# Count tables with an operand in PSUM, and the last combines divided between VectorE and GpSimd, in an attention and mixture-of-experts kernel

## The chip, the cores and the metric

The kernel runs as one program on one core of a Trainium2 chip. The metric is the device time of one execution in microseconds (us); lower is better. The engines are TensorE (PE in the rows, its weight loads PEld), VectorE (DVE), ScalarE (ACT), GpSimd (POOL) and SyncE (SP), each with an instruction stream of its own. A "q" behind an engine's name (ACTq, DVEq, POOLq) is its queue, which issues DMAs and handles registers and semaphores.

## What is computed

```python
scores = scale * np.matmul(q, k.transpose(0, 1, 3, 2))     # 2 x 8 heads, 768 tokens, 64 wide
keep = is_sink | in_window                                  # 4 sinks, window of 128
a = softmax(np.where(keep, scores, -1e9))
x = merge_heads(np.matmul(a, v))                            # 1536 tokens x 512
h = x @ w_in                                                # 512 x 2048
x = (h - np.tanh(h)) @ w_out                                # 2048 x 512
noisy = x @ w_gate + np.log1p(np.exp(x @ w_noise)) * noise  # 8 experts
for each token: the two experts with the highest noisy value, softmax of the two as weights
for e in range(8):
    out[mask] += weight * (np.maximum(x[mask] @ w1[e], 0.0) @ w2[e])   # 512 x 1024, 1024 x 512
```

All of it is float32. Every matmul of the three stages behind the attention is made of three: each operand is split into a high part rounded to fp32r and a low part, the remainder, and hi*hi + hi*lo + lo*hi are added up in PSUM.

## The kernel before, in words

**Stages.** The first 94 us or so are attention. Then four blocks of 384 tokens go through the dense layer, and VectorE computes the routing of each block while TensorE works on the next. A token's row is scattered by GpSimd (an indirect DMA) into `sorted_x`, grouped by expert. The expert stage then works on `TILES` = 31 tiles of 128 sorted rows, expert by expert. With these inputs 29 tiles hold rows; the last two are spare and are computed all the same.

**One tile of the expert stage.** TensorE's loop for tile t does `up(t)` (24 matmuls of 512 columns, L1598), `turn_rows(t + 1)` (four transposes of the next tile's rows, L1580) and `down(t - 2)` (24 matmuls, L1630). The hidden rows of a tile go by DMA to memory and back (`hid_out`, `hid_in`, L901 and L909, both issued by ScalarE) so that VectorE can transpose them in 32x32 blocks (`turn_hidden`, L1199). VectorE's loop does, for tile t: `relu_out(t)` (L1207), `rows_turned_out(t + 1)` (L1190, the low part of the next tile's turned rows), `turn_hidden(t - 1)`, `result_out(t - 2)` (L1214, the result from PSUM to `ys`), and `hid_turned_out(t - 1)` (L1220). ScalarE does `relu_out(t)`, `hid_out(t)`, the high part of the turned rows (L886), the load of rows t + 2, `hid_turned_out(t - 1)` (L922), `store_rows(t - 2)` (L926, `ys` to `sorted_y`) and `hid_in(t)`. The order is written out by hand. On each engine an instruction that waits holds up all behind it.

**The tables.** While the first tiles run, VectorE computes small tables from the counts of rows per expert. Each step is `link`ed: it is followed by a wait of VectorE for its own result. The tables are in the `arena` (SBUF) or, those called `..._t`, in bank 6 of PSUM. The last of them, `stores_i` (L1334 to L1345), tells GpSimd how many tiles must be stored before the rows of a block can be gathered. It stands between `hid_turned_out(2)` and the loop over tiles 4 to 28. It reads `placed`, the running counts after each block, which `route_place` writes (L1143).

**The weights.** SyncE loads the weights of an expert in four pieces into a ring of two slots, when TensorE is done with the expert that was there. GpSimd splits each piece into the high part (L656) and the low part (L658), 128 x 2048 elements per instruction.

**The end.** When all experts are split, GpSimd gathers for each of the 12 output tiles of 128 tokens first the rows of one expert (`gathered_a`), and scales them by the gate (L740), then those of the other expert (`gathered_b`). These are multiplied by their gate (L745) and added (L748) in `combine`. The first gather of each block of three tiles waits for the stores that it needs (L757 to L759); gather i waits for gather i - 3. SyncE stores each output tile when it is combined (L603), and waits at the end for these stores and for those of `sorted_y` (L606). On TensorE the last pieces are `down(29)` and `down(30)`; VectorE takes out result 29 (L1366), ScalarE result 30 (L986).

The waits behind which the last tiles' results stand:

```python
            for i in range(TT):
                sp.wait_ge(summed, i + 1)
                sp.dma_start(out[token(i):token(i) + P, :], gathered_a[:, i, :]).then_inc(out_stored, 16)
            sp.wait_ge(out_stored, 16 * TT)

            sp.wait_ge(ys_stored, 16 * TILES)
```

## Time and profile before

| | |
|---|---|
| median of 3 runs | 769.12 us (768.66 to 769.92) |
| the profiled execution's own time | 771.69 us |
| its span, first to last instruction | 769.9 us |
| granted TensorE clock, mean | 0.978 |
| TensorE matmul busy | 741.4 us (96%) |
| GpSimd busy | 464.2 us (60%) |
| VectorE busy | 364.6 us (47%) |
| ScalarE busy | 229.4 us (30%) |

Times in the rows are microseconds from the start of the span. The chain of waits follows the work that ended last back to its start. A clock of 1.00 is TensorE's full 2.4 GHz, 0.50 is 1.2 GHz.

### The profile page before, as it was taken

How to read it: one execution, taken by the hardware profiler on the slowest of the kernel's cores; microseconds unless marked ns; L12 is line 12 of the kernel's file. 1: busy time of each engine (PE TensorE's matmuls, PEld its weight loads, DVE VectorE, ACT ScalarE, POOL GpSimd, SP SyncE). 2: the span in 40 equal slices, each digit the busy share in tenths (PEclk: the TensorE clock that was granted, in tenths of full speed). 3: DMA queues.
4: the chain of work that ended last, by engine and by line, in shares of the span. 5: the costliest groups of instructions: out<-in, count | busy, mean ns of one | idle time of the engine just before them, and what ended most of it. 6: DMA issues, size and time to landing. Idle time of an engine off the chain costs nothing.

```text
span 769.9 us, 12878 instructions
## 1 busy us (share of the span) xinstructions
PE 741.4 (96%) x3892; PEld 622.4 (81%) x3893; DVE 364.6 (47%) x877; ACT 229.4 (30%) x528; POOL 464.2 (60%) x264
## 2 busy tenths in 40 slices
PE   7999999999999999999999699999999999999993
PEld 5777899898989998998877478888888888888882
DVE  4777544224423532353464854454454454455440
ACT  5999622223222322322221111211211211212220
POOL 6888997000300110038959936858885899987687
PEclk8999999999999999999899989999999999999997
DMA  8642483000200010025633548677776777867664
GB/s 298 231 139 92 144 314 150 0 1 1 83 1 0 14 68 0 0 73 186 238 146 107 179 152 260 216 235 261 241 247 214 249 256 246 257 192 247 225 199 150
DMA packets 59550, 121.46 MB, mean 158 GB/s; under 512 B 7040, under 2 KB 21504, under 8 KB 59520
## 3 DMA queue, kind: packets, MB, share of 16 engines
q1 hardware_dynamic: 28512, 63.92, 24.3%
q10 hardware_dynamic: 27168, 44.57, 17.2%
q0 software_dynamic: 3840, 12.59, 5.0%
q8 instruction: 16, 0.26, 0.1%
q14 instruction: 14, 0.11, 0.0%
HBM read 81.74 MB, written 39.32 MB: 157 GB/s over the span
## 4 chain that ended last, share of the span: by engine, by line
PE 90%; POOL 3%; DVE 2%; issue 1%; DMA 1%; ACT 1%; POOLq 0%; ACTq 0%; DVEq 0%
PE bank L1598 21%; PE bank L1630 20%; PE bank L1455 18%; PE bank L1505 18%; PE bank L1408 4%; PE bank L1399 3%; PE bank L1381 3%; PE bank L1580 2%; PE bank L1521 1%; POOL gathered_b L745 1%; POOL gathered_a L748 1%; POOL gathered_b L733 1%; PE bank L1515 1%; DMA hid_lanes<-hid_by_lane 1%; DVE arena L1334 0%
## 5 line engine op out<-in xcount | busy, mean ns | idle before, releaser
L704 POOL DMA_INDIRECT sorted_x<-y_rows,arena x24 | 24.2, 1010 | 208.9 <-DVEq L1142 202.8
L658 POOL TENSOR_TENSOR ring<-ring_raw,ring 128x2048 fp32r<-128x2048 f32 x32 | 148.0, 4624 | 2.5
L1630 PE MATMUL bank<-ring,hidT_hi 128*128 (+1 forms) x464 | 148.2, 400 | 1.0 <-DVE hidT_lo L1220 1.0
L656 POOL TENSOR_TENSOR ring<-ring_raw,ones 128x2048 fp32r<-128x2048 f32 x32 | 115.9, 3622 | 54.3 <-DMA ring_raw<-in_moe_w 54.3
L1598 PE MATMUL bank<-ring,xsT_hi 128*128 (+1 forms) x496 | 137.8, 401 | 10.8 <-DVE xsT_lo L1190 8.8
L1598 PEld LDWEIGHTS bank<-ring,xsT_hi 128*128 128x128 f32 x496 | 95.5, 194 | 32.8 <-issue 12.2
L1505 PE MATMUL bank<-w_out_sb,gated_hi 128*128 128x512 f32 x384 | 121.2, 397 | 0.0
L1630 PEld LDWEIGHTS bank<-ring,hidT_hi 128*128 128x128 f32 x464 | 84.9, 188 | 19.6 <-issue 1.2
L1630 PE MATMUL bank<-ring,hidT_lo 128*128 (+1 forms) x232 | 91.6, 395 | 0.0
L1063 DVE TENSOR_TENSOR arena<-bank,arena 128x384 f32<-128x384 f32 x64 | 35.7, 557 | 113.7 <-ACT arena L835 112.7
L1455 PE MATMUL bank<-xT_hi,w_in_hi 128*128 (+1 forms) x256 | 87.0, 340 | 0.0
L1455 PE MATMUL bank<-xT_hi,w_in_lo 128*128 (+1 forms) x256 | 86.4, 338 | 0.0
L1455 PE MATMUL bank<-xT_lo,w_in_hi 128*128 (+1 forms) x256 | 86.0, 336 | 0.0
L1505 PEld LDWEIGHTS bank<-w_out_sb,gated_hi 128*128 128x128 f32 x384 | 70.9, 188 | 12.3
L1598 PE MATMUL bank<-ring,xsT_lo 128*128 (+1 forms) x248 | 78.4, 398 | 0.0
L1505 PE MATMUL bank<-w_out_sb,gated_lo 128*128 128x512 f32 x192 | 75.9, 395 | 0.0
L835 ACT ACTIVATE arena<-bank 128x384 f32<-128x384 f32 x64 | 31.4, 491 | 139.8 <-PE bank L1455 139.8
L1207 DVE TENSOR_SCALAR hid<-bank 128x512 f32<-128x512 f32 x31 | 21.4, 691 | 97.3 <-PE bank L1598 97.3
L922 ACT CAST hidT_hi<-bank 128x512 fp32r<-128x512 f32 x58 | 31.5, 590 | 117.9 <-PE bank L1630 97.5
L1199 DVE STREAM_TRANSPOSE bank<-hid_lanes 128x512 f32<-128x512 f32 x56 | 64.5, 1197 | 2.2 <-DMA hid_lanes<-hid_by_lane 2.2
L1067 DVE TENSOR_TENSOR gated_lo<-arena,gated_hi 128x384 fp32r<-128x384 f32 x64 | 45.8, 716 | 40.0 <-ACT gated_hi L840 40.0
L1598 PEld LDWEIGHTS bank<-ring,xsT_lo 128*128 128x128 f32 x248 | 47.7, 192 | 10.4
(201 smaller groups left out, 1074.1 us busy)
## 6 DMA issues: line engine op xcount, KB each, us to landing
ring_raw<-in_moe_w SPq DMA_DIRECT2D x48, 512.0 KB, 4.2
hid_by_lane<-hid ACTq DMA_DIRECT2D x28, 512.0 KB, 3.4
hid_lanes<-hid_by_lane ACTq DMA_DIRECT2D x28, 512.0 KB, 4.5
ring_raw<-in_moe_w SPq DMA_DIRECT2D x8, 1024.0 KB, 7.0
sorted_y<-ys ACTq DMA_DIRECT2D x31, 256.0 KB, 2.6
xs<-sorted_x ACTq DMA_DIRECT2D x27, 256.0 KB, 3.7
sorted_y<-zeros SPq DMA_DIRECT2D x1, 4864.0 KB, 25.5
arena<-in_k SPq DMA_DIRECT2D x8, 520.0 KB, 4.1
```

The source lines that it names most:

```text
L656: pool.tensor_tensor(hi, raw, one_like(raw), ALU.mult).then_inc(rounded, 1)
L658: ins = pool.tensor_tensor(lo, raw, hi.bitcast(F32), ALU.subtract)
L835: act.activation(tanh_h[fc % 2][:, :], bank[fc % 2][:, 0:BLK], ACT.Tanh).then_inc(tanh_ready, 1)
L922: act.copy(hidT_hi[b][:, half * BANK:(half + 1) * BANK], bank[3 + half][:, :]).then_inc(hidT_rounded, 1)
L1063: dve.tensor_tensor(gated[fc % 2][:, :], bank[fc % 2][:, 0:BLK], tanh_h[fc % 2][:, :], ALU.subtract).then_inc(gated_ready, 1)
L1067: dve.tensor_tensor(gated_lo[fc % G][:, :], gated[fc % 2][:, :], gated_hi[fc % G][:, :].bitcast(F32), ALU.subtract).then_inc(gated_split, 1)
L1199: dve.transpose(bank[3 + half][:, :].rearrange("p (c i g) -> p g c i", c=EC // 2, g=QUAD), lane_blocks[:, :, half * (EC // 2):(half + 1) * ...
L1408: last = pe.matmul(attn_bank[half][D * u:D * u + D, at:at + w], lhs, rhs, start=start, stop=stop, skip_group_check=True)
L1455: last = pe.matmul(bank[fc % 2][:, 0:BLK], w[:, at:at + P], x[:, bass.ds(blk * CH + c, 1), :].rearrange("p a s -> p (a s)"), start=c == 0 ...
L1505: last = pe.matmul(bank[2 + kk][:, :], g[fc % G][:, kk * P:(kk + 1) * P], w_out_sb[:, fc, w, :], start=fc == 0 and n == 0, stop=fc == FC - ...
L1598: last = pe.matmul(bank[1 + half][:, :], x[:, c * P:(c + 1) * P], ring[:, bass.ds(at * 2 * WE + (w + c * FE + half * BANK), BANK)], start= ...
L1630: last = pe.matmul(bank[5 + b][:, :], x[:, c * P:(c + 1) * P], ring[:, bass.ds(at * 2 * WE + (w + CH * FE + c * DM), DM)], start=c == 0 an ...
```

## The change

It has three parts.

1. **The table of stores.** `placed` is first copied into PSUM (`placed_all_t`). `placed_d`, and `placed_end`, lie in PSUM now (`placed_d_t`, `placed_end_t`). So no instruction of this table reads two operands from SBUF, and none goes from SBUF to SBUF with a single operand. In `route_place`, `placed` is written by an addition with an operand in PSUM, three instructions earlier than the copy that it replaces.
2. **The last combines.** GpSimd combines output tiles 0 to 5. VectorE combines tiles 6 to 11, behind all its other work, with one instruction for each (multiply by the gate and add). SyncE waits for a new semaphore for these six. GpSimd still issues all the gathers.
3. **The last results.** ScalarE takes out result 29 as well as result 30.

```diff
+    LATE = 2 * KB
...
             for i in range(TT):
-                sp.wait_ge(summed, i + 1)
+                if i < TT - LATE:
+                    sp.wait_ge(summed, i + 1)
+                else:
+                    sp.wait_ge(last_summed, i + 1 - (TT - LATE))
...
                     for i in range(blk * KB, blk * KB + KB):
                         gather(kk, rows, i)
-                        if i >= 2:
-                            finish(i - 2)
-                for i in range(TT - 2, TT):
-                    finish(i)
+                        if kk == 0 and i >= 2:
+                            scale(i - 2)
+                        if kk == 1 and 2 <= i < TT - LATE + 2:
+                            combine(i - 2)
+                if kk == 0:
+                    scale(TT - 2)
+                    scale(TT - 1)
...
             hid_turned_out(TILES - 1, used=TILES - 1, b=1)
+            result_out(TILES - 2)
             store_rows(TILES - 2)
 
-            act.wait_ge(expert_done, TILES + 1)
-            act.wait_ge(ys_stored, 16 * (TILES - 1))
-            act.copy(ys[:, :], bank[6][:, :]).then_inc(ys_ready, 1)
+            result_out(TILES - 1, b=1)
             store_rows(TILES - 1)
...
+                dve.tensor_tensor(placed[:, bass.ds(blk, 1), :].rearrange("p b e -> p (b e)"), carry[:, KB - 1, :],
+                                  bank[7][:, 2 * P + (KB - 1) * E:2 * P + KB * E], ALU.add)
                 link(dve.tensor_tensor(row_t, rank_t, carry[:, 0:KB, :], ALU.add))
...
-                dve.tensor_copy(placed[:, bass.ds(blk, 1), :].rearrange("p b e -> p (b e)"), carry[:, KB, :])
                 link(dve.tensor_copy(carry[:, 0, :], carry[:, KB, :]))
...
-            link(dve.tensor_tensor(placed_swap[:, :, :], placed[:, :, :],
+            link(dve.tensor_copy(placed_all_t, placed[:, :, :]))
+            link(dve.tensor_tensor(placed_swap[:, :, :], placed_all_t,
                                    swap[:, None, :].to_broadcast([P, NBLK, E]), ALU.mult))
-            link(dve.tensor_reduce(placed_d[:, :], placed_swap[:, :, :], AX.X, ALU.add))
+            link(dve.tensor_reduce(placed_d_t, placed_swap[:, :, :], AX.X, ALU.add))
             link(dve.tensor_tensor(placed_at_t, swap[:, None, E - TOP:E].to_broadcast([P, NBLK, TOP]),
-                                   placed_d[:, :, None].to_broadcast([P, NBLK, TOP]), ALU.mult))
+                                   placed_d_t[:, :, None].to_broadcast([P, NBLK, TOP]), ALU.mult))
...
-            link(dve.tensor_tensor(placed_end[:, :, :], placed_tiles[:, :, :],
+            link(dve.tensor_tensor(placed_end_t, placed_tiles[:, :, :],
                                    tile_end_t[:, None, E - TOP - 1:E - 1].to_broadcast([P, NBLK, TOP]), ALU.add))
-            dve.tensor_scalar(stores_i[:, :, :], placed_end[:, :, :], 16.0, None, ALU.mult).then_inc(stores_known, 1)
+            dve.tensor_scalar(stores_i[:, :, :], placed_end_t, 16.0, None, ALU.mult).then_inc(stores_known, 1)
...
             hid_turned_out(TILES - 1, 1)
-            result_out(TILES - 2)
+
+
+            for i in range(TT - LATE, TT):
+                dve.wait_ge(gathered[1][i], 16)
+                dve.wait_ge(scaled, i + 1)
+                dve.scalar_tensor_tensor(gathered_a[:, i, :], gathered_b[:, i, :], gate_at[1][:, i:i + 1],
+                                         gathered_a[:, i, :], ALU.mult, ALU.add).then_inc(last_summed, 1)
```

Two places show how the instructions stand. The first is on VectorE, between the split of tile 2's turned hidden rows and the loop; `arena` is SBUF, `bank` is PSUM. Before:

```order
L1220 TENSOR_TENSOR hidT_lo<-bank,hidT_hi 128x512 x2
L1334 TENSOR_TENSOR arena<-arena 128x32
L1336 TENSOR_REDUCE arena<-arena 128x4
L1337 TENSOR_TENSOR bank<-arena 128x8
L1339 TENSOR_TENSOR bank<-arena,bank 128x8
L1340 TENSOR_SCALAR bank<-bank 128x8
L1341 TENSOR_SCALAR bank<-bank 128x8
L1342 CAST arena<-bank 128x8
L1343 TENSOR_TENSOR arena<-arena,bank 128x8
L1345 TENSOR_SCALAR arena<-arena 128x8
```

With the change:

```order
L1235 TENSOR_TENSOR hidT_lo<-bank,hidT_hi 128x512 x2
L1349 COPY bank<-arena 128x32
L1350 TENSOR_TENSOR arena<-bank,arena 128x32
L1352 TENSOR_REDUCE bank<-arena 128x4
L1353 TENSOR_TENSOR bank<-arena,bank 128x8
L1355 TENSOR_TENSOR bank<-arena,bank 128x8
L1356 TENSOR_SCALAR bank<-bank 128x8
L1357 TENSOR_SCALAR bank<-bank 128x8
L1358 CAST arena<-bank 128x8
L1359 TENSOR_TENSOR bank<-arena,bank 128x8
L1361 TENSOR_SCALAR arena<-bank 128x8
```

Nine instructions became ten, and in the three that had `arena` alone on both sides (L1334, L1337 and L1345) a `bank` stands now.

The second is on GpSimd at its end: the combine of output tile 4, then that of 5, with the last gathers. Before, the last rows of GpSimd are:

```order
L733 DMA gathered_b<-sorted_y,arena 128x512
L745 TENSOR_TENSOR gathered_b<-gathered_b,arena 128x512
L748 TENSOR_TENSOR gathered_a<-gathered_a,gathered_b 128x512
L745 TENSOR_TENSOR gathered_b<-gathered_b,arena 128x512
L748 TENSOR_TENSOR gathered_a<-gathered_a,gathered_b 128x512
L745 TENSOR_TENSOR gathered_b<-gathered_b,arena 128x512
L748 TENSOR_TENSOR gathered_a<-gathered_a,gathered_b 128x512
L76 UNCONDITIONAL_BRANCH
```

With the change:

```order
L751 TENSOR_TENSOR gathered_b<-gathered_b,arena 128x512
L754 TENSOR_TENSOR gathered_a<-gathered_a,gathered_b 128x512
L739 DMA gathered_b<-sorted_y,arena 128x512
L763 TENSOR_LOAD arena
L763 ISA x2
L739 DMA gathered_b<-sorted_y,arena 128x512 x3
L77 UNCONDITIONAL_BRANCH
```

The gathers of tiles 8 to 11 now follow one another, and twelve instructions of GpSimd (two for each of six tiles) are gone. In their place `L1387 SCALAR_TENSOR_TENSOR` stands six times at VectorE's end.

## Rows read from the trace of the kernel before

**Rows 1.** First lines of the page: the span.
```profile
span 769.9 us, 12878 instructions
```

**Rows 2.** Waits of PE from 440 us on: total, times, longest us.
```profile
PE bank L1598 <- DVE xsT_lo L1190: 8.4, 1, 8.4
```

**Rows 3.** Chain of waits, around 440 us: start us, us, what.
```profile
438.12 3.06 issue
...
443.97 8.52 PE bank L1598 x24
...
458.52 5.45 PE bank L1598 x24
```

**Rows 4.** DVE's timeline, 416 to 442 us: start, us, line, op, out<-in.
```profile
416.19 0.16 DVE L1314 TENSOR_SCALAR bank<-arena 128x12 f32<-128x12 f32 x1
...
429.26 3.89 DVE L1334 TENSOR_TENSOR arena<-arena 128x32 f32<-128x32 f32 x1
...
433.41 3.29 DVE L1337 TENSOR_TENSOR bank<-arena 128x8 f32<-128x8 f32 x1
...
437.75 3.52 DVE L1345 TENSOR_SCALAR arena<-arena 128x8 int32<-128x8 f32 x1
```

**Rows 5.** POOL's timeline, 412 to 476 us.
```profile
412.05 4.58 POOL L658 TENSOR_TENSOR ring<-ring_raw,ring 128x2048 fp32r<-128x2048 f32 x1
...
428.51 4.59 POOL L658 TENSOR_TENSOR ring<-ring_raw,ring 128x2048 fp32r<-128x2048 f32 x1
433.06 3.60 POOL L656 TENSOR_TENSOR ring<-ring_raw,ones 128x2048 fp32r<-128x2048 f32 x1
436.74 4.49 POOL L658 TENSOR_TENSOR ring<-ring_raw,ring 128x2048 fp32r<-128x2048 f32 x1
...
467.35 3.60 POOL L656 TENSOR_TENSOR ring<-ring_raw,ones 128x2048 fp32r<-128x2048 f32 x1 [17.88 <-DMA ring_raw<-in_moe_w]
```

**Rows 6.** Windows: us; PE, PEld, DVE, ACT, POOL busy (x); PEclk, DMA share, GB/s.
```profile
445.00:450.00 5.00, 5.00 (x13) 3.93 (x12) 2.62 (x4) 1.06 (x2) 4.46 (x1) 0.51 0.65 197
450.00:455.00 5.00, 5.00 (x25) 4.10 (x24) 1.09 (x2) 1.19 (x2) 0.00 (x0) 1.00 0.15 52
```

**Rows 7.** L909 (`hid_in`): the one of 429.0 us, then four from 415 to 470 us.
```profile
L909 ACTq DMA_DIRECT2D hid_lanes<-hid_by_lane x1: 326/326/326, 429.0 to 429.0; - x1
...
DMA to landing us min/median/max: 4.4/4.4/4.4
...
DMA to landing us min/median/max: 3.6/4.5/5.1
```

**Rows 8.** POOL's timeline from 716 us to its end.
```profile
717.55 0.95 POOL L733 DMA_INDIRECT gathered_b<-sorted_y,arena  x1 [0.30 <-issue]
...
739.73 0.99 POOL L733 DMA_INDIRECT gathered_b<-sorted_y,arena  x1 [1.81 <-DMA sorted_y<-ys]
...
743.31 0.99 POOL L733 DMA_INDIRECT gathered_b<-sorted_y,arena  x1
...
764.40 1.26 POOL L748 TENSOR_TENSOR gathered_a<-gathered_a,gathered_b 128x512 f32<-128x512 f32 x1
```

**Rows 9.** Landing times by line: L603 (12), L926 from 690 us (7), L733 from 700 us (17).
```profile
DMA to landing us min/median/max: 2.0/2.0/3.8
...
DMA to landing us min/median/max: 2.1/3.0/3.8
...
DMA to landing us min/median/max: 3.4/3.6/6.0
```

**Rows 10.** ACT's timeline at its end.
```profile
757.76 0.59 ACT L986 COPY ys<-bank 128x512 f32<-128x512 f32 x1 [6.97 <-PE bank L1630]
758.38 0.34 ACTq L926 DMA_DIRECT2D sorted_y<-ys  x1
```

**Rows 11.** DVE's timeline at its end.
```profile
750.34 1.29 DVE L1220 TENSOR_TENSOR hidT_lo_last<-bank,hidT_hi_last 128x512 fp32r<-128x512 f32 x2 [3.93 <-ACT hidT_hi_last L922]
```

**Rows 12.** L1067 by itself, two SBUF operands: duration ns min/median/max.
```profile
L1067 DVE TENSOR_TENSOR gated_lo<-arena,gated_hi x64: 557/559/1829, 93.3 to 369.3; 128x384 fp32r<-128x384 f32 x64
```

More of the change, by code:

```diff
@@ L265, in build @@
         placed_swap = part([NBLK, E])
-        placed_d = part([NBLK])
         placed_tiles = part([NBLK, TOP])
-        placed_end = part([NBLK, TOP])
         filled = part([E])
@@ L320, in build @@
         gate_last_t = [table([TT]) for k in range(TOP)]
+        placed_all_t = table([NBLK, E])
+        placed_d_t = table([NBLK])
         placed_at_t = table([NBLK, TOP])
+        placed_end_t = table([NBLK, TOP])
         placed_t = table([NBLK, TOP])
@@ L431, in build @@
         summed = sem("summed")
+        last_summed = sem("last_summed")
         out_stored = sem("out_stored")
@@ L754, in _ @@
             pool.wait_ge(gates_ready, 2)
-            for kk, rows, finish in ((0, gathered_a, scale), (1, gathered_b, combine)):
+            for kk, rows in ((0, gathered_a), (1, gathered_b)):
                 for blk in range(NBLK):
@@ L922, in hid_turned_out, with result_out @@
                     act.copy(hidT_hi[b][:, half * BANK:(half + 1) * BANK], bank[3 + half][:, :]).then_inc(hidT_rounded, 1)
+            def result_out(t, b=0):
+                act.wait_ge(expert_done, t + 2)
+                act.wait_ge(ys_stored, 16 * t)
+                act.copy(ys[:, :], bank[5 + b][:, :]).then_inc(ys_ready, 1)
             def store_rows(t):
```

## The prediction

> **What bounds the kernel now.** I began with the page: TensorE is busy for nearly the whole of a span of 769.9 us [rows 1]. So only two things can pay: a place where TensorE stands still, and what is left when TensorE is done. I looked for the first in TensorE's waits. From 440 us on there is a single one, 8.4 us long, for the low part of the turned rows, which VectorE makes [rows 2]. The chain of waits shows this place: between 438.12 and 443.97 us it runs over VectorE and ScalarE, and the `up(5)` behind it takes 8.52 us where the next takes 5.45 [rows 3]. The windows say why the first is longer: TensorE's granted clock is 0.51 there and 1.00 in the next five microseconds [rows 6]. So the pause costs twice, as a pause and as a stretch at the lower level, 1.2 GHz.
>
> Why VectorE is late is in its timeline. Three tiny instructions take 3.89, 3.29 and 3.52 us [rows 4]. Laid beside GpSimd's timeline they end where GpSimd's instructions end: 433.15 against 433.10, 436.70 against 436.66, 441.27 against 441.23 us [rows 4, 5]. They wait for GpSimd's splits of the weights. All three have no operand in PSUM on the reading side. A table step of the same kind from SBUF into PSUM took 0.16 us at 416.19 us, in the middle of a GpSimd split (412.05 to 416.63) [rows 4, 5]. So a place in PSUM does free a step.
>
> The end of the program hangs on another engine. TensorE ends at about 757.7 us, just ahead of ScalarE's copy of the last result [rows 10]. GpSimd is at work until 765.66 us [rows 8], the last store of the output is issued right behind it and lands 2.0 us later, at 767.7 [rows 9], and 2.2 us after that the span ends. GpSimd has one gather and two arithmetic steps for each output tile, a period of 3.58 us (739.73 to 743.31) [rows 8].
>
> **Part 1, the table.** Its ten steps have an operand in PSUM each. Taking 0.16 us and the issue of the next, some 0.2 us for each, they take about 2.1 us, so from 429.35 the table is done at 431.5 instead of 441.2 us. That is no longer what is last. Late next is the landing of `hid_in(3)`: it was issued at 429.0 and took 4.4 us [rows 7], to 433.4 us, and ScalarE must see it before `hid_out(4)`, behind which the high part of the turned rows is queued. From there to TensorE the trace has these steps: 0.5 us for the issue, 0.6 for ScalarE's copy, 0.7 for VectorE's subtraction, 0.15 to TensorE, about 2.0 in all: TensorE could go on at 435.4 us. `down(2)` ends at 435.5. So the pause goes to 0 or little more. TensorE saves 8.45 us of pause (435.52 to 443.97) and 8.52 - 5.45 = 3.07 us of slow clock: **11.5 us**. The bounds of this term: `hid_in` took 3.6 to 5.1 us near here [rows 7], so up to 0.7 us of pause may stay; nothing in the rows gives more than 11.5.
>
> What could eat it is the weights. GpSimd is busy with the third expert's first pieces until 449.5 us; `up(8)` needs them and comes at 470 us instead of 481. The next piece starts at 467.35 after an idle 17.88 us, waiting for a load [rows 5] which in turn waits for TensorE, so it moves forward with it. The cover is 20 us, and I cost it at nothing. In `route_place` one instruction of 0.1 us comes ahead of the scatter in each of four blocks and one goes behind it. Three are beside TensorE's dense layer, and the fourth may delay the first scatter of the last block by 0.1 us: nothing.
>
> **Parts 2 and 3, the end.** In times of the trace before (all of it moves 11.5 us forward): GpSimd's gather of tile 6 stays at 739.73 us, since it waits for a store of tile 27 [rows 8]. With combines 4 and 5 in between, gather 8 comes at 746.9. Then there is no arithmetic. Gathers with nothing in between follow at 1.25 us (717.55 and its neighbours) [rows 8], with 0.6 us for reading the table once, so gather 11 is issued at about 751.2 and lands 3.4 to 3.6 us later [rows 9], at 754.7.
>
> VectorE is done with its own work at 751.63 us [rows 11]; the copy of result 29 is ScalarE's now, which has been idle there. Six combines follow. The trace has none, so their price is an estimate. A pair of VectorE instructions over 512 columns takes 1.29 us, 0.65 each [rows 11], and one over 384 columns with both operands in SBUF takes 0.56 us [rows 12], in proportion 0.74 for 512. I take 0.65 us from one to the next, as in the pair, 3.9 us in all (4.5 by the other row), so the last ends at about 755.6 us, and its store has landed at about 757.7. That is **ahead of** the last result, and with this the end passes to TensorE: copy at 757.76, store at 758.38 us [rows 10], landing, 2.2 us of closing. The landing is the open price: 2.1 to 3.8 us [rows 9]. The 3.8 is of this same store, with the last gather and output stores beside it; in the changed kernel these are over. So I take 2.1, the quiet end: 758.4 + 2.1 + 2.2 = 762.7 instead of 769.9, **7.2 us**; with 3.8 it is 5.5.
>
> The upper bound of a combine: if a second operand from SBUF doubled the time of each column, a step would take 1.2 us instead of 0.65. Six are 7.2 us, from 751.63 to 758.8; the store lands at 760.9 and the span ends at 763.1 instead of 762.7. The one row with two SBUF operands, 0.56 us for 384 columns, speaks against it, but that is an instruction with one operation, and these have two [rows 12].
>
> The Trainium skill has this as a rule, on the page "Vector Engine (DVE) Microarchitecture Reference", section "Points that are easy to get wrong": a scalar_tensor_tensor with two sources in SBUF that aren't bf16 runs at half throughput. By it the end would be 763.1, not 762.7 us, and the forecast 750.8; no row shows the instruction at this size.
>
> **Sum.** 11.5 + 7.2 = 18.7 us. The profiled execution has 771.69 us of its own, 1.8 over its span, and would have 753.0. It lies 2.6 us over the median of the runs, 769.12, so for the runs I forecast 769.12 - 18.7 = **750.4 us**.
>
> **The rivals.**
>
> - A, the forecast (70%): both ends as above; its own range is 749.0 to 752.2, from 0.7 us of pause that stays, the landing of 3.8 us, and the spread of the runs.
> - B (10%): a pause of more than a microsecond stays at 435 us since `hid_in` lands later or ScalarE and VectorE, pushed together, get in each other's way. For it speaks that the margin is only 0.1 us. One of 2 us costs 2 and perhaps the slow clock's 3.07 again: up to 755.5.
> - C (10%): VectorE's combines end last, since each takes 1.2 us (750.8 us, above), or since they wait for GpSimd's gathers as the table's steps did for the splits. A gather keeps GpSimd for 1 us, and only the last of them lies behind 751 us: 1 us on top, 751.8.
> - D (5%): one of the waits stays, because the new copy out of SBUF waits as L1345 did. It would hold until 433.1 us, the table would end at 435, TensorE would go on at about 437.8: 2.3 us, or 5.3 with the slow clock, so 752.7 to 755.7. Against it is the step of 416.19 us [rows 4].
> - E (3%): a part does not do what it says. Without the first the time is 761.9, without the second 757.6 us.
> - F (2%), slower than before: TensorE's clock. The change takes away its one pause in 320 us. If the chip answered unbroken work with its lower level, every microsecond of work would cost one more. It decides against the change when over 20 us of work, 40 us of time, run at 0.50: 18.7 are then lost and 1.5 more, 770.7 us and above. Against it: the clock was low after the pause and full in long unbroken work [rows 6].
>
> **How the numbers follow.** A measurement here can tell 0.2% (1.5 us) from no change. A to E are all faster than before by more, F is slower; I leave 0.01 for no difference. The range takes A, C, and the nearer halves of B and D: 748.5 to 754.5 us.
>
> **What would show it.** After 429 us: table steps of some 0.2 us, no wait of TensorE for `xsT_lo`, `up(5)` in about 5.5 us at a clock of 1.00. At the end: six combines on VectorE of 0.65 to 0.75 us (1.2 if halved), GpSimd done before TensorE, the last thing to land a store into `sorted_y`, 4.3 us or so between its issue and the end of the span. The forecast is wrong if TensorE shows a new wait behind 435 us, for rows or for weights, or if an output store is the last to land.

## The result and the profile after

The changed kernel took **747.02 us** in the median of 4 runs (744.54 to 748.84), beside 769.52 (768.66 to 772.89) for the kernel before. The ratio is 0.9698, with a 95% interval of 0.9656 to 0.9739: 22.5 us faster, where 18.7 were forecast. The time is 1.5 us under the lower end of the forecast range. The profiled execution took 744.54 us, with a span of 742.8 instead of 769.9 [rows 1], so the pair of profiles differs by 27.1 us. It is the fastest of its four, while that of before lay 2.6 us over the median. How much of the difference belongs to the two executions, and not to the two kernels, is a question for the experiments.

Rows of the page of after: the span, busy times, the granted clock in 40 slices (the gain of the last two rows is told below):

```profile
span 742.8 us, 12879 instructions
PE 729.9 (98%) x3892; PEld 617.5 (83%) x3893; DVE 355.3 (48%) x883; ACT 230.0 (31%) x529; POOL 451.0 (61%) x252
PEclk9999999999999999999999999999999999999999
L1652 PE MATMUL bank<-ring,hidT_hi 128*128 (+1 forms) x464 | 145.9, 395 | 1.4 <-DVE hidT_lo L1235 1.0
L1652 PE MATMUL bank<-ring,hidT_lo 128*128 (+1 forms) x232 | 90.7, 391 | 0.0
```

**The table.** VectorE's timeline of after, from 425 us (columns as in [rows 4]):

```profile
425.51 0.18 DVE L1349 COPY bank<-arena 128x32 f32<-128x32 f32 x1
...
427.41 0.17 DVE L1361 TENSOR_SCALAR arena<-bank 128x8 int32<-128x8 f32 x1
427.71 0.69 DVE L1222 TENSOR_SCALAR hid<-bank 128x512 f32<-128x512 f32 x1
430.20 0.69 DVE L1205 TENSOR_TENSOR xsT_lo<-bank,xsT_hi 128x512 fp32r<-128x512 f32 x1 [1.80 <-ACT xsT_hi L895]
```

GpSimd's and ScalarE's, the same stretch:

```profile
425.35 4.62 POOL L664 TENSOR_TENSOR ring<-ring_raw,ring 128x2048 fp32r<-128x2048 f32 x1
```
```profile
429.10 0.38 ACTq L910 DMA_DIRECT2D hid_by_lane<-hid  x1
429.58 0.59 ACT L895 CAST xsT_hi<-bank 128x512 fp32r<-128x512 f32 x1 [2.95 <-DMA hid_lanes<-hid_by_lane]
```

The ten steps take 2.07 us (425.51 to 427.58), in the middle of a split of GpSimd (425.35 to 429.97). Before, three of nine took 3.89, 3.29 and 3.52 us [rows 4]. What is late next is the landing of `hid_in(3)`: ScalarE stands 2.95 us for it. The chain of after shows that this costs nothing:

```profile
426.43 5.47 PE bank L1652 x24
431.90 5.44 PE bank L1620 x24
438.14 5.73 PE bank L1652 x24
```

`up(5)` begins where `down(2)` ends and takes 5.44 us, where it came 8.45 us late and took 8.52 us before [rows 3]. The windows show the clock at its upper level there, 2.4 GHz:

```profile
431.00:437.00 6.00, 6.00 (x28) 4.95 (x28) 3.80 (x5) 1.18 (x2) 5.92 (x2) 1.00 0.86 289
```

**The end.** GpSimd, VectorE and ScalarE in their timelines, then SyncE's waits, all of after:

```profile
730.89 0.95 POOL L739 DMA_INDIRECT gathered_b<-sorted_y,arena  x1 [0.30 <-issue]
733.00 0.96 POOL L739 DMA_INDIRECT gathered_b<-sorted_y,arena  x1 [1.16 <-DMA gathered_b<-sorted_y,arena]
```
```profile
731.95 1.29 DVE L1235 TENSOR_TENSOR hidT_lo_last<-bank,hidT_hi_last 128x512 fp32r<-128x512 f32 x2 [3.83 <-ACT hidT_hi_last L931]
733.15 4.26 DVE L1387 SCALAR_TENSOR_TENSOR gathered_a<-gathered_b,arena,gathered_a 128x512 f32<-128x512 f32 x6
```
```profile
739.24 0.59 ACT L937 COPY ys<-bank 128x512 f32<-128x512 f32 x1 [4.85 <-PE bank L1652]
739.85 0.34 ACTq L941 DMA_DIRECT2D sorted_y<-ys  x1
```
```profile
SPq L612 <- DMA sorted_y<-ys: 4.2, 1, 4.2
SPq L77 <- PEq L77: 0.2, 1, 0.2
```

Six combines take 4.26 us together and end at 737.4 us, before TensorE does. The last thing to land is a store into `sorted_y`, 2.5 us behind its issue at 739.85, and 0.4 us later the span ends. From TensorE's end to the end of the span it is 3.6 us, where it was 12.2 (757.7 to 769.9).

**Where the 27.1 us of this pair are.** Pause and slow clock: 8.45 + 3.08 = 11.5. The end: 12.2 - 3.6 = 8.6. `up(0)`, the first of the expert stage: 8.30 us before, 5.59 after, 2.7, and 0.5 more in the 16 small matmuls just ahead of it (2.37 and 1.85 us). Of the change only an addition of 0.1 us for each block in `route_place` lies ahead of these, and two more profiles of the kernel before, below, have an `up(0)` of 5.60 and of 8.12 us, so this part belongs to the executions. And something that the prediction doesn't have: each later `down` takes 5.47 to 5.49 us instead of 5.60, and each `up` some 0.02 us less. From the end of `up(5)` to TensorE's end it is 301.85 us instead of 305.23, 3.4. Together 26.7.

### The profile page after: what moved, and what is told of

Read it like the earlier page. It is cut to its first block, busy times and chain, and to the rows that moved or that the text cites. A ratio compares the mean times of both kernels' runs of the same rounds, so it can differ in the third digit from the quotient of the medians.

```text
span 742.8 us, 12879 instructions
## 1 busy us (share of the span) xinstructions
PE 729.9 (98%) x3892; PEld 617.5 (83%) x3893; DVE 355.3 (48%) x883; ACT 230.0 (31%) x529; POOL 451.0 (61%) x252
## 3 DMA queue, kind: packets, MB, share of 16 engines
q10 hardware_dynamic: 27168, 44.57, 17.9%
## 4 chain that ended last, share of the span: by engine, by line
PE 97%; ACT 1%; DVE 1%; POOL 1%; issue 0%; POOLq 0%; ACTq 0%; DVEq 0%
PE bank L1652 23%; PE bank L1620 23%; PE bank L1477 18%; PE bank L1527 18%; PE bank L1430 4%; PE bank L1421 3%; PE bank L1403 3%; PE bank L1602 2%; PE bank L1543 1%; PE bank L1537 1%; ACT arena L789 1%; PE bank L1486 1%; POOL arena L686 0%; DVE hid L1222 0%; PE bank L1630 0%
## 5 line engine op out<-in xcount | busy, mean ns | idle before, releaser
L1652 PE MATMUL bank<-ring,hidT_hi 128*128 (+1 forms) x464 | 145.9, 395 | 1.4 <-DVE hidT_lo L1235 1.0
L1620 PE MATMUL bank<-ring,xsT_hi 128*128 (+1 forms) x496 | 133.3, 390 | 2.3 <-DVE hid L1222 2.0
L1620 PEld LDWEIGHTS bank<-ring,xsT_hi 128*128 128x128 f32 x496 | 92.7, 188 | 22.3 <-issue 3.3
L1620 PE MATMUL bank<-ring,xsT_lo 128*128 (+1 forms) x248 | 76.5, 390 | 0.0
L1081 DVE TENSOR_TENSOR gated_lo<-arena,gated_hi 128x384 fp32r<-128x384 f32 x64 | 45.7, 714 | 40.0 <-ACT gated_hi L849 40.0
L1214 DVE STREAM_TRANSPOSE bank<-hid_lanes 128x512 f32<-128x512 f32 x56 | 62.0, 1151 | 2.3 <-DMA hid_lanes<-hid_by_lane 2.3
L923 ACT ACTIVATE hid<-bank 128x512 f32<-128x512 f32 x31 | 18.6, 600 | 119.9 <-PE bank L1620 119.9
```

The source lines that it names most:

```text
L1081: dve.tensor_tensor(gated_lo[fc % G][:, :], gated[fc % 2][:, :], gated_hi[fc % G][:, :].bitcast(F32), ALU.subtract).then_inc(gated_split, 1)
L1214: dve.transpose(bank[3 + half][:, :].rearrange("p (c i g) -> p g c i", c=EC // 2, g=QUAD), lane_blocks[:, :, half * (EC // 2):(half + 1) * ...
L1620: last = pe.matmul(bank[1 + half][:, :], x[:, c * P:(c + 1) * P], ring[:, bass.ds(at * 2 * WE + (w + c * FE + half * BANK), BANK)], start= ...
L1652: last = pe.matmul(bank[5 + b][:, :], x[:, c * P:(c + 1) * P], ring[:, bass.ds(at * 2 * WE + (w + CH * FE + c * DM), DM)], start=c == 0 an ...
```

## The experiments

Each group shares one chip and the runs of the kernel before on it. The theories: **(1)** the forecast's sum, 11.5 and 7.2; **(2)** the faster `down` comes from the place of its stationary operand, the turned hidden rows. `placed_d` and `placed_end`, 16 columns ahead of the hidden rows, have left the arena, so `hidT_hi` and `hidT_lo` lie 64 bytes lower (with `hid_lanes` and some small tables); rival: it comes from timing at the table or at the end. **(3)** The rest of 22.5 - 18.7 is in how executions differ.

### First group: one part at a time

The kernel before with the two small tables allotted behind the hidden tiles, and nothing else:

```diff
-        placed_d = part([NBLK])
         placed_tiles = part([NBLK, TOP])
-        placed_end = part([NBLK, TOP])
...
         assert FE == 2 * DM
+        placed_d = part([NBLK])
+        placed_end = part([NBLK, TOP])
```

> The kernel before, with only the place of data changed: two small tables are allotted behind the turned hidden rows instead of ahead of them, so hidT_hi, hidT_lo and hid_lanes lie 16 columns (64 bytes) lower in SBUF, where the changed kernel has them. The changed kernel's 24 matmuls of a down take 5.47 us where those of before take 5.60. If that is due to the place, down takes 5.45 to 5.47 us here too, and 27 of them give 3 to 4 us less than before, with the pause at 435 us still there. If it is due to anything else in the change, or to the chip's state in that run, down stays at 5.60 us and the time within 1 us of before.

Measured: 765.04 us (12 executions, 759.4 to 768.8) beside 767.18 (21); ratio 0.9955 (0.9922 to 0.9987), by which it is 3.5 us (1.0 to 6.0) faster; the medians lie 2.1 us apart. The chain and the page of this kernel:

```profile
507.72 5.47 PE bank L1630 x24
...
L1630 PE MATMUL bank<-ring,hidT_hi 128*128 (+1 forms) x464 | 145.9, 395 | 1.0 <-DVE hidT_lo L1220 1.0
```

The rate of the changed kernel is there (5.47 us, 395 ns a matmul on the page) with no instruction changed; the pause is there too (8.7 us).

The changed kernel with 16 unused columns in the tables' old place:

```diff
+        part([16])
         placed_tiles = part([NBLK, TOP])
```

> The changed kernel with 16 unused columns ahead of the turned hidden rows, so that they lie where the kernel before has them. If the place sets the rate, down takes 5.60 us again and the time is 3 to 4 us over that of the changed kernel (750 to 751 us, which is what was forecast). If it does not, nothing changes.

Measured: 750.84 us (6; 748.3 to 752.4); ratio 0.9781 (0.9740 to 0.9822). Its chain and page:

```profile
509.15 5.60 PE bank L1653 x24
...
L1653 PE MATMUL bank<-ring,hidT_hi 128*128 (+1 forms) x464 | 148.2, 400 | 1.1 <-DVE hidT_lo L1236 1.0
```

So the slower rate comes back with the place alone, and without the pause. Theory 2 holds for the rate, in both directions, and its rival falls. The time of this version, 750.84 us, tells less: no set of the changed kernel stands beside it on this chip, and on the other chips that kernel measured 746.5 to 750.6.

Part 1 of the change alone, the small tables' places kept:

```diff
-            link(dve.tensor_tensor(placed_swap[:, :, :], placed[:, :, :],
+            link(dve.tensor_copy(placed_all_t, placed[:, :, :]))
+            link(dve.tensor_tensor(placed_swap[:, :, :], placed_all_t,
...
-            dve.tensor_scalar(stores_i[:, :, :], placed_end[:, :, :], 16.0, None, ALU.mult).then_inc(stores_known, 1)
+            dve.tensor_scalar(stores_i[:, :, :], placed_end_t, 16.0, None, ALU.mult).then_inc(stores_known, 1)
```

> The kernel before with the first part alone: the table of stores has an operand in PSUM, no data moves in SBUF, the combines and the last results are as before. If the pause and the slow clock behind it hang on VectorE's three waits for GpSimd, TensorE has no pause at 435 us, up(5) takes 5.5 us, and the time is 10.8 to 11.5 us under before. If the three waits only hid another wait, a pause of over 1 us is left.

Measured: 759.60 us (8; 756.6 to 762.1); ratio 0.9906 (0.9870 to 0.9943), 7.2 us (4.4 to 10.0). No pause, `down` 5.60 us. The mechanism is as forecast; 11.5 us lies outside the interval, and so do the 10.8 to 11.5 that were expected here.

Parts 2 and 3 alone:

```diff
-                        if i >= 2:
-                            finish(i - 2)
+                        if kk == 1 and 2 <= i < TT - LATE + 2:
+                            combine(i - 2)
...
-            result_out(TILES - 2)
+            for i in range(TT - LATE, TT):
+                dve.wait_ge(gathered[1][i], 16)
```

> The kernel before with the second and third part alone, the table with its three waits as before and no data moved. From TensorE's end to the end of the span: 12.2 us before, 3.6 us in the changed kernel. If these two parts alone do this, the time is 8 to 9 us under before (7.2 was forecast), and the pause of 8.4 us at 435 is there. If the closing of 2.2 us behind the last landing is not tied to these parts, the gain is 6 to 7.5 us.

Measured: 760.38 us (8; 756.9 to 763.3); ratio 0.9906 (0.9870 to 0.9943), again 7.2 us (4.4 to 10.0). The pause is there (8.6 us). From TensorE's last matmul to the end of the span it is 3.1 us (757.8 to 760.9). The time gains less than the 8 to 9 us that were expected from this. The three pieces make 7.2 + 7.2 + 3.5 = 17.9 us by the ratios (7.6, 6.8 and 2.1 by the medians).

### Second group: which place is fast

The arena's allotment gives the byte at which each tile begins in a partition. The weights that `down` streams (`ring`) begin at 96 modulo 128; `hidT_hi` begins at 32 before the change and at 96 after it. Two more places, by 8 and by 24 columns of padding:

```diff
+        part([8])
         placed_tiles = part([NBLK, TOP])
```

> The changed kernel with the turned hidden rows 8 columns (32 bytes) higher, at 0 modulo 128 bytes. If only the same place modulo 128 as the streamed weights (96) is fast, down takes 5.60 us; if the slow place is the one of before (32) alone, it takes 5.47.

> The same with 24 columns (96 bytes), at 64 modulo 128 bytes. Down takes 5.60 us if only 96 is fast, 5.47 if 32 alone is slow. Together with the run at 0 this maps the four places that the allocation allows.

Measured, one execution each: 748.17 and 755.24 us. `down` in the chain of the one with 8 columns (0 modulo 128), then of the one with 24 (64 modulo 128):

```profile
506.87 5.61 PE bank L1653 x24
```
```profile
501.42 5.61 PE bank L1653 x24
```

At 0, 32 and 64 it takes 5.59 to 5.62 us, at 96 alone 5.47 to 5.49. `up`, whose stationary operand `xsT` lies at 96 by the same allotment in all versions, takes 5.44 to 5.48 us in all of them. Whether what counts is the 96 or that it equals the streamed operand's place can't be told, since `ring` was never moved.

The gated rows, stationary operand of the dense layer's second matmuls, begin at 64. Moved to 96 in the changed kernel:

```diff
         behind_routing = used[0]
+        part([8])
```

> The changed kernel with 8 unused columns (32 bytes) ahead of gated_hi and gated_lo, the operands of the dense layer's second matmul. Byte addresses modulo 128: the weights and rows that the matmuls stream in (w_out, ring) lie at 96; hidT lay at 32 before (5.60 us for 24 matmuls) and lies at 96 now (5.47); gated lies at 64 and would lie at 96. Nine of its matmuls take 2.10 us, 233 ns each, as in the slow case of down. If it is the place against the streamed operand that sets the rate, nine take 2.04 us and 64 groups of nine give 3.5 to 4 us less than the changed kernel. If the dense layer is bound otherwise, 2.10 stays and the time too.

Measured: 750.68 us (6; 748.9 to 751.6), ratio 0.9799 (0.9768 to 0.9831). Nine matmuls take 2.08 instead of 2.10 us, 27 take 6.16 instead of 6.30: a gain of the same sign, smaller than for the nine that were expected in 2.04. The total was no better, and the profile shows why: TensorE waits 3.9 us for `gated_lo`, which it did in none of the profiles so far but that with 24 columns (3.4 us).

The changed kernel again, unchanged, to see if that wait belongs to the move:

> The changed kernel once more, unaltered, beside the others of this call on one chip. The first measurement was 747.02 us (744.5 to 748.8), with the profiled run the fastest of four. The sum of the parts run one by one against before (table 7.6 us, end 6.8, moved data 2.1) is 16.5 us; the terms read in the traces (11.2, 8.6, 3.6) give 23.4. The run tells which of the two the change is worth, about 750.7 or about 744 us.

Measured: 750.63 us (6; 744.5 to 755.1), ratio 0.9786 (0.9741 to 0.9832), and the same wait in the very kernel that had none in its first profile. L1081 (`gated_lo`, two operands in SBUF) in this execution's VectorE timeline, and GpSimd's splits beside it:

```profile
349.22 3.94 DVE L1081 TENSOR_TENSOR gated_lo<-arena,gated_hi 128x384 fp32r<-128x384 f32 x1 [0.64 <-ACT gated_hi L849]
354.27 3.79 DVE L1081 TENSOR_TENSOR gated_lo<-arena,gated_hi 128x384 fp32r<-128x384 f32 x1 [0.63 <-ACT gated_hi L849]
...
371.82 3.73 DVE L1081 TENSOR_TENSOR gated_lo<-arena,gated_hi 128x384 fp32r<-128x384 f32 x1 [0.64 <-ACT gated_hi L849]
```
```profile
349.16 3.60 POOL L662 TENSOR_TENSOR ring<-ring_raw,ones 128x2048 fp32r<-128x2048 f32 x1 [2.91 <-DMA ring_raw<-in_moe_w]
352.83 4.81 POOL L664 TENSOR_TENSOR ring<-ring_raw,ring 128x2048 fp32r<-128x2048 f32 x1
```

The same two in the first profile of the changed kernel:

```profile
348.25 0.56 DVE L1081 TENSOR_TENSOR gated_lo<-arena,gated_hi 128x384 fp32r<-128x384 f32 x1 [0.63 <-ACT gated_hi L849]
...
369.29 1.43 DVE L1081 TENSOR_TENSOR gated_lo<-arena,gated_hi 128x384 fp32r<-128x384 f32 x1 [0.64 <-ACT gated_hi L849]
```
```profile
349.18 3.60 POOL L662 TENSOR_TENSOR ring<-ring_raw,ones 128x2048 fp32r<-128x2048 f32 x1 [2.45 <-DMA ring_raw<-in_moe_w]
```

GpSimd starts at the same microsecond in both (349.16, 349.18). In the first profile the step of 348.25 is over before it; in the second VectorE is 1 us later, its step starts just behind GpSimd's, and ends 0.40 us behind GpSimd's end (353.16, 352.76). From then on each step waits for one of GpSimd's instructions, six in a row, until TensorE runs out of rows, and its clock falls behind that. The windows of this execution:

```profile
370.00:380.00 10.00, 6.78 (x26) 5.36 (x27) 5.60 (x4) 2.23 (x4) 9.84 (x4) 0.85 0.22 81
380.00:390.00 10.00, 9.82 (x47) 8.35 (x46) 5.61 (x29) 2.61 (x6) 3.60 (x1) 0.67 0.95 343
```

It is the wait of part 1 at another place, in one execution and not in the next. What makes VectorE late is ScalarE: its tanh, for which VectorE waits, starts 1 us later, though TensorE's matmuls ahead of it are not late. It comes at 347.51 us instead of 346.54, and TensorE's last matmul ahead of it begins at 346.08 us instead of 346.16.

Why ScalarE starts late no row says. And being late is not enough: in four other profiles, two of them of the kernel before, the step came at 349.0 to 349.2 us and still 0.1 to 0.5 us ahead of GpSimd's first split, and nothing waited. In the four profiles with the six waits it began 0.05 to 0.24 us behind that split's start.

### Third group: how executions differ, and a version that goes round the wait

The kernel before, unchanged, for one more profile:

> The kernel before, unaltered, a second profile. In the first, TensorE's clock was at 0.51 behind the pause (up(5) 8.52 us) and also in up(0) (8.30 us), and that execution was 2.6 us over the median. Three of four profiles of kernels with the change's tail on another chip state (e6, e7, e8) show VectorE's last six gated_lo steps of the dense layer waiting 2.8 to 3.9 us each for GpSimd's splits, about 5 us in all; the first profile of before shows none. If both are events that come and go with the execution, this profile may differ from the first at 344 to 384 us by 0 to 8 us, in a kernel that is the same to the instruction.

Measured: 763.65 us. The table on VectorE, and GpSimd beside it:

```profile
425.00 0.18 DVE L1334 TENSOR_TENSOR arena<-arena 128x32 f32<-128x32 f32 x1
...
425.43 4.39 DVE L1337 TENSOR_TENSOR bank<-arena 128x8 f32<-128x8 f32 x1
...
430.88 2.50 DVE L1345 TENSOR_SCALAR arena<-arena 128x8 int32<-128x8 f32 x1
```
```profile
425.20 4.58 POOL L658 TENSOR_TENSOR ring<-ring_raw,ring 128x2048 fp32r<-128x2048 f32 x1
```

L1334 began 0.20 us before a split of GpSimd's and took 0.18 us; in the profile of [rows 4] it began 0.75 us behind one's start and took 3.89. Two waits are left of three, TensorE's pause is 3.7 us instead of 8.45, and `up(5)` takes 8.57 us: 6.8 in all instead of 11.5. The reduction L1336 between them, from SBUF to SBUF as well, doesn't wait; in the profile of [rows 4] it began at 433.19 us, 0.13 behind the start of a split, and took 0.19.

The step where `gated_lo` takes its second operand from the PSUM bank instead of an SBUF tile, on top of the gated rows at 96. The difference h - tanh(h) stays in its bank, and TensorE waits for the split before it reuses the bank:

```diff
-                dve.tensor_tensor(gated[fc % 2][:, :], bank[fc % 2][:, 0:BLK], tanh_h[fc % 2][:, :],
+                dve.tensor_tensor(bank[fc % 2][:, 0:BLK], bank[fc % 2][:, 0:BLK], tanh_h[fc % 2][:, :],
...
-                dve.tensor_tensor(gated_lo[fc % G][:, :], gated[fc % 2][:, :], gated_hi[fc % G][:, :].bitcast(F32),
+                dve.tensor_tensor(gated_lo[fc % G][:, :], bank[fc % 2][:, 0:BLK], gated_hi[fc % G][:, :].bitcast(F32),
...
-                    pe.wait_ge(gated_ready, blk * FC + fc - 1)
+                    pe.wait_ge(gated_split, blk * FC + fc - 1)
```

> e7 (the changed kernel, gated_hi and gated_lo 8 columns higher) with one more edit: VectorE writes h - tanh(h) back into the PSUM bank that h came from, ScalarE rounds it from there, and VectorE's gated_lo subtraction reads it there, so it has one operand in SBUF instead of two. TensorE waits for gated_split instead of gated_ready before it writes the bank again, some 1.2 us later with 3 us and more to spare. If these steps wait for GpSimd in part of the executions, all gated_lo steps now take 0.56 us, no wait of TensorE for gated_lo is left, the median is 3 to 5 us under e8's 750.63 and e7's 750.68, and the spread (744.5 to 755.1) becomes narrower. If the spread comes from the clock alone, the median stays at about 749.

Measured: 744.79 us (6; 742.8 to 747.3); ratio 0.9712 (0.9672 to 0.9752). VectorE's groups from 340 to 378 us in this kernel:

```profile
L1082 DVE TENSOR_TENSOR gated_lo<-bank,gated_hi 128x384 fp32r<-128x384 f32 x7 | 3.9, 558 | 4.2 <-ACT gated_hi L850 4.2
```

The mean is 558 ns, where it is 2750 for the same stretch in the profile with the waits and 1014 in the first of after. That this version is faster than the changed kernel isn't shown by this set alone, which has no set of that kernel on its chip.

The closing: the changed kernel where GpSimd waits for TensorE's end and then has two more instructions (fills of a constant that nothing reads any more), to see if 2.2 or 0.4 us goes with GpSimd's end:

```diff
+            pool.wait_ge(expert_done, TILES + 1)
+            for u in range(2):
+                pool.memset(zeros[:, u * DM // 2:(u + 1) * DM // 2], 0.0)
```

> The changed kernel with GpSimd kept at work to the end: behind its last gather it waits for TensorE's last matmul and then fills 512 columns of an unused constant. From GpSimd's end to the end of the span it was 4.2 us before, with the last landing in between; from the last landing to the end 2.2 us before and 0.4 with the change. If the closing is long because GpSimd is done late, GpSimd's end at about 740.3 (on the clock of the first profile) gives an end at 744.5, 2 us behind the last landing. If it depends on which DMA lands last, the end stays 0.4 us behind the landing of the last store into sorted_y.

Measured: 751.46 us, one execution; `up(0)` took 8.4 us in it. GpSimd's last row, then SyncE's last waits:

```profile
744.93 0.56 POOL L777 MEMSET zeros<- 128x256 f32 x2 [4.53 <-PE bank L1655]
```
```profile
SPq L612 <- DMA sorted_y<-ys: 3.5, 1, 3.5
SPq L77 <- PEq L77: 0.9, 1, 0.9
```

GpSimd ends at 745.5 us and the span 4.2 us later, at 749.7. Before the change it was 765.66 and 769.9, 4.2 as well, and in the other profiles with GpSimd's combines last (three versions, two more of the kernel before) it is 4.2 to 4.3. The last wait, for TensorE's queue, grows from 0.2 to 0.9 us; in the six profiles with GpSimd's combines last it is 2.0. So all profiles fit a span that ends by the later of two: 4.2 us behind GpSimd's last instruction, or some 0.4 behind the last landing. The one run that moved GpSimd's end shows this with a shift of 0.7 us in one execution, not with the 2 us that were expected. What fills the 4.2 us no row says.

One wait put back into the changed kernel, L1345's:

```diff
-            link(dve.tensor_tensor(placed_end_t, placed_tiles[:, :, :],
+            link(dve.tensor_tensor(placed_end[:, :, :], placed_tiles[:, :, :],
...
-            dve.tensor_scalar(stores_i[:, :, :], placed_end_t, 16.0, None, ALU.mult).then_inc(stores_known, 1)
+            dve.tensor_scalar(stores_i[:, :, :], placed_end[:, :, :], 16.0, None, ALU.mult).then_inc(stores_known, 1)
```

> The changed kernel with placed_end back in SBUF, so that the last step of the table (L1345 before) goes from SBUF to SBUF again and the two others keep their operand in PSUM. On the first profile of the changed kernel it would start at 427.4 us, in a GpSimd split that ends at 429.97. If each such step waits to the end of the GpSimd instruction in course, it takes 2.5 to 3.5 us, VectorE's relu_out(4) comes at about 430.0 instead of 427.7, and TensorE, which went on at 431.90 without a pause, stands still for 0.7 to 1.5 us, since ScalarE and VectorE need some 2.7 us from there to the low part of the turned rows. If one such wait is hidden by the landing of the hidden rows, there is no pause.

Measured: 745.61 us, one execution. VectorE and GpSimd:

```profile
427.09 2.79 DVE L1362 TENSOR_SCALAR arena<-arena 128x8 int32<-128x8 f32 x1
```
```profile
425.26 4.60 POOL L665 TENSOR_TENSOR ring<-ring_raw,ring 128x2048 fp32r<-128x2048 f32 x1
```

The step that takes 0.17 us from a bank takes 2.79 from SBUF and ends with GpSimd's (429.88, 429.86). TensorE waits 0.8 us for `xsT_lo` and `up(5)` takes 5.74: one wait of three costs 1.1 us, since `hid_in` lands late anyway.

### Fourth and fifth group: the changed kernel and the PSUM operand, side by side

The changed kernel, a third time:

> The changed kernel unaltered, a third time, as the control of the three others of this call. 747.0 us and 750.6 us so far, single executions from 744.5 to 755.1. If executions differ by VectorE's six late gated_lo steps, a profile of 743 to 745 us has gated_lo at 0.56 to 1.8 us and one of 748 us and more has them at 2.8 to 3.9.

The changed kernel with the PSUM operand for `gated_lo` alone, the gated rows in their old place:

> The changed kernel with only the PSUM operand for gated_lo, gated left in its place in SBUF (e10 had both). If the waits of gated_lo for GpSimd are what costs, this is 3 to 6 us under e13 on the same chip, with a range of executions no wider than 5 us; the 8 columns of e10 are worth 1 us at most (9 matmuls 2.08 instead of 2.10 us, 64 times). If e10's 744.79 was the chip's or the place's doing, it is within 1.5 us of e13.

The kernel before with the same step alone:

> The kernel before with the same edit of gated_lo. If the late gated_lo steps cost the kernel before as often as the changed one, it is 3 to 6 us under before. If in before the order of GpSimd's and VectorE's instructions falls well by itself (both profiles of before have no gated_lo over 2.1 us), it is within 1.5 us of before.

And the kernel before for one more profile:

> A third profile of the kernel before. The first (own time 771.69) had three waits in the table and a pause of 8.4 us, the second (763.65) two, 4.4 and 2.5 us, and a pause of 3.7 us; the slow clock behind it cost 3.1 us in both. If the pause follows where the table falls in GpSimd's row of 3.6 and 4.6 us instructions, it is between 3 and 9 us here, and the pause and the clock in up(0) account for most of the difference in time.

Measured: 746.45 (6; 743.8 to 748.7), 747.21 (6; 744.2 to 749.9), 767.99 (12; 761.3 to 770.8) and 767.21 us (one), beside 765.18 for the kernel before (17). The ratios are 0.9743 (0.9707 to 0.9778), 0.9758 (0.9722 to 0.9794) and 1.0021 (0.9988 to 1.0054). The PSUM operand alone gained nothing in either kernel. For the changed one this is a miss, since 3 to 6 us had been expected if the waits cost time; for the kernel before it is the second of the two outcomes that were put down. The profile of the changed kernel had no waits in `gated_lo` this time (mean 993 ns, 2750 with them), so there was nothing to gain in it. The last profile of before has two waits (L1337 and L1345, 4.32 and 2.50 us), a pause of 3.9 us, and an `up(0)` of 8.12.

Then the PSUM operand with the gated rows at 96 once more, and beside it on the same chip the changed kernel a fourth time:

> e10 again (gated_hi and gated_lo 8 columns higher, gated_lo with its operand in PSUM), now beside the changed kernel on one chip. e10 measured 744.79 us, 2.9% under its before; the changed kernel 747.0, 750.6 and 746.5. Nine matmuls of the dense layer take 2.08 us for 2.10, which is worth 64 x 0.02 = 1.3 us. If that is all, it is 0 to 3 us under e18; if e10 was a version clearly better, 4 us and more.

> The changed kernel unaltered, control of e17 and a fourth measurement: 744 to 751 us. The pooled difference to before is 19.7 us so far (747.1 against 766.8); forecast were 18.7. If the first measurement's 22.5 us was chance on both sides, the ratio here lies at 0.972 to 0.979.

Measured: 744.34 us (6; 743.5 to 746.0) and 750.38 (6; 744.7 to 755.5), beside 765.87 for the kernel before (11). The ratios are 0.9718 (0.9678 to 0.9757) and 0.9781 (0.9734 to 0.9828). The changed kernel's profile, that of its slowest execution, has the waits in `gated_lo` again: the chain leaves TensorE for it.

```profile
373.48 3.74 DVE gated_lo L1081
...
386.64 8.34 PE bank L1620 x24
```

In the other kernel the chain stays on TensorE: the 27 matmuls at the end of the dense layer start at 366.25 us, and `up(0)` takes 5.60.

```profile
366.25 6.17 PE bank L1528 x27
...
377.48 5.60 PE bank L1621 x24
```

**This version beats both kernels**: 744.8 and 744.3 us in two sets of six, on two chips, with the changed kernel at 750.4 beside the second. Neither of its two edits alone was faster than the changed kernel beside it (750.68 and 750.63 us, 747.21 and 746.45), so which of them gives how much is not shown. Two things of it are seen in the profiles: the faster place saves 1.2 us by the last block (366.25 against 367.43 in the kernel with the PSUM operand alone), and the waits in `gated_lo` are gone, which where they happened held TensorE for 3.4 to 3.9 us, with a slow clock behind it in the second group's and this one's.

## Why the prediction was right or wrong

**The whole.** Over all its executions the changed kernel has a median of 748.2 us (22; 743.8 to 755.5), the kernel before 766.7 (77; 761.6 to 773.0). That is 18.5 us, and 18.7 had been forecast. But the match is luck: over all executions one term was too large and one was missing, and these two nearly cancel. In the first pair of sets, 22.5 us apart, they did not: its traces have the 11.5 us of part 1 as forecast, and on top the missing term (3.4), a shorter closing (1.4 with the landing) and `up(0)` (3.2 with the matmuls ahead of it). And the time of the kernel before stood 2.4 us too high. The forecast was taken from a median of three runs, 769.12; from 766.7 the same sum would give 748.0. The set of the kernel before on that chip is the slowest of six (769.52 against 765.2 to 767.2); whether that is the chip or chance isn't known. The measured 747.02 is within the spread of the kernel itself. A range from 748.5 up was too narrow for a kernel whose own executions span 12 us.

**Part 1, mechanism: right.** The steps of the table wait for GpSimd's splits, an operand in PSUM frees them (0.17 to 0.20 us each), `hid_in(3)` is late next, and TensorE doesn't wait. The Trainium skill, page "SBUF — State Buffer", section "Who interferes with whom", has VectorE's second port pair shared with GpSimd under an exclusive lock. The traces agree: the tensor_tensor steps with both operands in SBUF, and the tensor_scalar step from SBUF to SBUF, end with GpSimd's instruction (at most 0.05 us behind it in the table, some 0.4 in `gated_lo`) or begin before it. The prediction's sign for a step that waits, no operand in PSUM on the reading side, is too wide: the reduction L1336 has none either and took 0.19 us just behind a split's start.

**The steps that failed.** Two steps of the sum "11.5 + 7.2 = 18.7 us" were wrong, in opposite directions: the size of its first term, and a term for the matmul rate that isn't in it.

**Part 1, size: too large.** The first is "TensorE saves 8.45 us of pause (435.52 to 443.97) and 8.52 - 5.45 = 3.07 us of slow clock". That was true of that execution alone, and the part's own experiment gave 7.2 (4.4 to 10.0). All three waits happened in it. Five more profiles have the old table: in three the pause was 8.2 to 8.7 us, in the two of the kernel before itself (763.65 and 767.21 us) it was 3.7 and 3.9, with two waits. The slow clock behind the pause cost 1.9 to 3.1 us. Pause and clock together are 5.8 to 11.6 us in the six profiles, 9.6 in the mean. So 11.5 stands at the upper end. The mean of 9.6 is within the experiment's interval; whether the part is worth 7.2 or 9.6 us stays open.

**Parts 2 and 3: right in kind, a little too small.** GpSimd's last gather, VectorE's combines and the last store came in the forecast order. The sum had 7.2 us; the pair of traces has 8.6, and the experiment 7.2 (4.4 to 10.0). The landing was 2.5 us, not 2.1. The closing was 0.4 us, not 2.2: "2.2 us of closing" was read behind the landing of the last store, but belongs to GpSimd's end, 4.2 us ahead of the end of the span. With GpSimd done at 734.0 us it is gone.

**What was missing.** The sum has nothing for the addresses: the prediction weighed what the change does to instructions, queues and weights, and not that data moves. Two small tables leave the arena and everything behind them moves by 64 bytes. `down` then takes 5.47 to 5.49 us instead of 5.60, shown in both directions; in time this is worth 3.5 us (1.0 to 6.0), shown in one.

**The rivals.** C, by which each combine takes 1.2 us, is refuted: 0.74 to 0.75 us in all profiles and 0.66 to 0.70 from one start to the next, with both operands in SBUF and float32. The rule of the Trainium skill beside it (page "Vector Engine (DVE) Microarchitecture Reference", section "Points that are easy to get wrong"), half throughput for two sources in SBUF that aren't bf16, does not show at this size: a step over the same 128x512 with one SBUF source takes 0.69 us, and half throughput would be twice that. In two profiles (the changed kernel's third set and the one with the gated rows at 96) the last gather lands late, and then an output store is the last to land, as this rival has it but by another cause. SyncE's waits in the former:

```profile
SPq L612 <- DMA sorted_y<-ys: 1.1, 1, 1.1
SPq L77 <- DMA out<-gathered_a: 1.0, 1, 1.0
```

The gather landed up to 5.5 us after its issue there, and it costs about 1 us. B, D and E did not happen. D's price, 2.3 us or more, is for a wait of the first step and wasn't run; with the last step waiting it was 1.1. F did not happen: without the pause TensorE's clock is 0.90 or more in every slice of the page of after.

**What stays open.** What makes ScalarE, and VectorE behind it, 1 us late ahead of `gated_lo`. Whether the change itself makes those six waits more frequent: four of the eleven profiles with the new table and `gated_lo` from SBUF have them, none of the five with the old table, too few to tell; if it does, they cost the change several us that no term has. What sets the clock in `up(0)`, which took 5.6 us in some executions and 6.9 to 8.4 in others, with either table. And what the 4.2 us behind GpSimd's end are.

## What to carry to other kernels

A pause that comes from two engines meeting is a property of the execution: take two or three profiles before pricing it, and put the operand in PSUM where a VectorE step with two SBUF operands waits for long GpSimd instructions in some of them. Where none waits, the move gains nothing. When a change adds or removes a tile, compare the addresses of what lies behind it, not only the instructions. And read the closing of a program from the engine that ends last, not as a constant.

## What the runs showed that was not expected

- **The place of the stationary operand changes the matmul rate.** With the streamed weights at 96 modulo 128 bytes, 24 matmuls of 512 columns take 5.47 to 5.49 us with the stationary operand at 96, and 5.59 to 5.62 at 0, 32 and 64. Nine of the dense layer's take 2.08 at 96 and 2.10 at 64, 27 take 6.16 to 6.17 and 6.30.
- **A wait between VectorE and GpSimd can lock in.** Six steps in a row of 0.56 us took 2.77 to 3.94 us each, since every one of them ended behind a GpSimd instruction and the next began inside the following one. What decided it was whether the first of them began behind the start of GpSimd's split (by 0.05 to 0.24 us) or ahead of it.
- **A tiny step just ahead of a GpSimd instruction is free**, and behind its start it waits for the rest of it: 0.18 against 3.89 us for the same 128x32 step with two SBUF operands.
- **The closing hangs on GpSimd:** the span ended 4.2 to 4.3 us behind GpSimd's last instruction wherever that came late, and otherwise 0.4 us behind the last landing.
